# Attention with rotary embedding, then a gated MLP, on one core: new orders of work for the five engines, two buffers for v, and a rope table loaded in halves

## What is computed

```
q_rot, k_rot = rotate(q), rotate(k)          # x1*cos - x2*sin, x1*sin + x2*cos
scores = (1/sqrt(64)) * q_rot @ k_rot.T      # 576 x 576 for each of 32 heads
attn = exp(scores - max) / (sum + 1e-9)
x = attn @ v                                 # 2304 x 512 over all heads
h = x @ w_in                                 # 2304 x 2048
g = h * tanh(log1p(exp(min(h, 20))))
y = g @ w_out                                # 2304 x 512
```

## Time and profile before

| what | value |
|---|---|
| median of three runs | 646.28 us (643.45 to 646.46) |
| the profiled execution's own time | 643.55 us |
| its span (first to last instruction) | 641.8 us |
| busy in the span: PE, ACT, DVE, POOL | 95%, 67%, 52%, 40% |
| Vt of the last pair, the end of attention on PE | from 241.70 us for 0.72 us |
| mean granted TensorE clock | 0.995 of full speed |

### The profile page before, as it was taken

The page is one execution under the profiler, slowest core; times in us unless marked ns, Lnnn a source line. Parts: engine busy times, 40 slices in busy tenths (PEclk is TensorE's granted clock), DMA queues, the critical chain, the costliest instruction groups (busy, mean ns, idle before and its releaser), DMA issues.

```text
span 641.8 us, 12510 instructions
## 1 busy us (share of the span) xinstructions
PE 610.3 (95%) x4484; PEld 467.2 (73%) x4484; DVE 331.4 (52%) x541; ACT 429.4 (67%) x693; POOL 259.6 (40%) x210
## 2 busy tenths in 40 slices
PE   0699999999999989999999999999999999999998
PEld 0366666666666658978888888888888888888886
DVE  1567777677778763864433335333534335234331
ACT  1567878788787766575865748675488575586663
POOL 3976778777878346996000431000620006000000
PEclk9989999999999989999999999999999999999999
DMA  6757786677777625050000051000330000000001
GB/s 217 206 168 195 212 239 198 187 221 222 209 204 197 168 63 151 1 131 34 0 1 1 0 132 66 1 0 2 93 103 0 0 0 0 33 33 0 0 0 65
DMA packets 39343, 60.20 MB, mean 94 GB/s; under 512 B 4880, under 2 KB 25104, under 8 KB 39184
## 3 DMA queue, kind: packets, MB, share of 16 engines
q1 hardware_dynamic: 39312, 59.79, 31.9%
HBM read 43.19 MB, written 9.51 MB: 82 GB/s over the span
## 4 chain that ended last, share of the span: by engine, by line
PE 82%; POOL 7%; DMA 5%; SPq 3%; issue 1%; DVE 1%; ACT 1%; ACTq 0%; POOLq 0%; DVEq 0%
PE ps_s L639 10%; PE ps_y L809 10%; PE ps_y L810 10%; PE ps_y L811 10%; PE ps_t L715 10%; PE ps_h L785 9%; PE ps_h L786 9%; PE ps_h L787 9%; PE ps_t L667 5%; POOL raw L504 2%; DMA xb_l<-r_early 2%; PE ps_t L727 1%; DMA raw<-qk_in 1%; POOL wout_lo L581 1%; DMA v_st<-v_in 1%
## 5 line engine op out<-in xcount | busy, mean ns | idle before, releaser
L1103 DVE TENSOR_TENSOR h_sb<-h_sb,m_sb 128x1024 f32<-128x1024 f32 x36 | 56.4, 1568 | 145.5 <-ACT m_sb L956 145.5
L1022 DVE TENSOR_SCALAR_CACHE_REDUCE minus_s<-ps_s 128x576 f32<-128x576 f32 x144 | 105.3, 753 | 34.1 <-PE ps_s L639 31.9
L809 PE MATMUL ps_y<-wout_hi,gh 128*128 128x512 f32 x288 | 112.2, 390 | 1.5 <-POOL wout_lo L581 1.5
L810 PE MATMUL ps_y<-wout_lo,gh 128*128 128x512 f32 x288 | 112.1, 389 | 0.0
L811 PE MATMUL ps_y<-wout_hi,gl 128*128 128x512 f32 x288 | 112.1, 389 | 0.0
L639 PE MATMUL ps_s<-qk_b,qk_a 64*128 64x288 f32 (+1 forms) x320 | 95.2, 442 | 15.7 <-DMA qk_b<-qk_a 12.2
L876 ACT ACTIVATE prob<-minus_s,neg_max 128x576 f32<-128x576 f32 x128 | 98.2, 774 | 13.6 <-DVE minus_s L1022 13.3
L504 POOL TENSOR_TENSOR raw<-raw,rope_t 128x576 f32<-128x576 f32 x62 | 86.7, 1421 | 50.2 <-DMA raw<-qk_in 50.2
L785 PE MATMUL ps_h<-xb_h,win_hi 128*128 128x512 f32 x256 | 99.6, 389 | 0.0
L786 PE MATMUL ps_h<-xb_l,win_hi 128*128 128x512 f32 x256 | 99.6, 389 | 0.0
L787 PE MATMUL ps_h<-xb_h,win_lo 128*128 128x512 f32 x256 | 99.6, 389 | 0.0
(11 more groups left out here) (71 smaller groups left out, 1018.4 us busy)
## 6 DMA issues: line engine op xcount, KB each, us to landing
raw<-qk_in SPq DMA_DIRECT2D x32, 576.0 KB, 4.1
v_st<-v_in SPq DMA_DIRECT2D x32, 160.0 KB, 2.3
qk_b<-qk_a SPq DMA_DIRECT2D x32, 144.0 KB, 2.4
x_transposed<-xt SPq DMA_DIRECT2D x64, 72.0 KB, 2.1
y_out<-y_sb SPq DMA_DIRECT2D x18, 256.0 KB, 2.0
win_raw<-w_in SPq DMA_DIRECT2D x16, 256.0 KB, 4.4
wout_raw<-w_out SPq DMA_DIRECT2D x16, 256.0 KB, 4.5
x_raw<-x_transposed SPq DMA_DIRECT2D x4, 1024.0 KB, 5.6
```

The costliest lines, as they stand in the source:

```text
L809: nc.tensor.matmul(o, g_h, wout_hi[:, f, :], start=(f == 0), stop=False)
L810: nc.tensor.matmul(o, g_h, wout_lo[:, f, :], start=False, stop=False)
L1022: nc.vector.tensor_scalar(minus_s[:, ring(word)], ps_s[:, score_buf(word, m), :, 0:SIDE], -1.0, None, ALU.mult, ALU.min, accum_out=neg_max ...
L1103: nc.vector.tensor_tensor(h_sb[:, c % 2, :], h_sb[:, c % 2, :], m_sb[:, c % 2, :], ALU.mult).then_inc(g_mul, 1)
```

## The change

Five things change together.

1. The three lists of words are new. On PE the four V words stand apart, each between scores, ST comes behind S0b, and TQ and Vt stand last. ACT and DVE follow this order.
2. `TURN_PAIR`: G4 moves to the pair of banks of V, and G0a and G1a to the other.
3. v has two buffers, so `load_v` of pair n waits for Vt of pair n-2 only, and v of pair 0 is loaded before the first step.
4. The rope table is loaded in two DMAs, one for each head, and DVE waits for the first alone.
5. In POOL's step `rotate(1, n + 2)` moves ahead of `add_parts(0, n + 2)`. Because ST is now behind S3a, `add_parts(0, ...)` waits for ST of pair n instead of S3a.

```diff
-PE_STEP = "S0a ST V0- V1- G4- S1a G0b- S2a S3a G1b- V2- V3- S0b S1b TQ Vt- S2b S3b G0a G1a".split()
-ACT_STEP = "G4- S0a G0b- ST G1b- S1a S2a S3a Xa- Xb- TQ S0b G0a G1a S1b S2b S3b".split()
-DVE_STEP = "S0a ST G4- S1a G0b- S2a G1b- S3a S0b S1b TQ S2b S3b G0a G1a".split()
+PE_STEP = "S0a S1a G4- G0b- S2a V0- S3a S0b G1b- V1- ST S1b G0a V2- S2b G1a S3b V3- TQ Vt-".split()
+ACT_STEP = "G4- S0a G0b- S1a S2a G1b- S3a S0b G0a ST S1b G1a S2b S3b Xa- Xb- TQ".split()
+DVE_STEP = "S0a G4- S1a S2a G0b- S3a S0b G1b- ST G0a S1b S2b G1a S3b TQ".split()
...
-TURN_PAIR = {"V": 0, "G4-": 1, "G0b-": 1, "G1b-": 1, "TQ": 1, "G0a": 0, "G1a": 1}
+TURN_PAIR = {"V": 0, "G4-": 0, "G0b-": 1, "G1b-": 1, "G0a": 1, "G1a": 1, "TQ": 1}
...
-        v_st = sb1("v_st", [P, 2, NT, D])
+        v_st = sb1("v_st", [P, 2, 2, NT, D])
...
-            def load_v(e, p):
+            def load_v(e, p, m):
...
-                if due(p):
-                    sp.wait_ge(pv_done, p)
+                if due(p - 1):
+                    sp.wait_ge(pv_done, p - 1)
                     sp.sem_inc(sp_through, 1)
-                sp.dma_start(v_st[:, e, :, :], head).then_inc(v_loaded[e], 16)
+                sp.dma_start(v_st[:, m, e, :, :], head).then_inc(v_loaded[m][e], 16)
...
-                if real(n):
+                if real(n) and not (isinstance(n, int) and n == 0):
                     for e in range(2):
-                        load_v(e, n)
+                        load_v(e, n, m)
...
             load_raw(0, 0)
-            sp.dma_start(rope_t[:], rope).then_inc(rope_loaded, 16)
-            load_raw(1, 0)
+            for e in range(2):
+                sp.dma_start(rope_t[:, e], rope[:, e]).then_inc(rope_loaded[e], 16)
+                if e == 0:
+                    load_raw(1, 0)
...
             load_raw(1, 1)
+            for e in range(2):
+                load_v(e, 0, 0)
...
                 if real(n + 2):
+                    rotate(1, n + 2)
                     add_parts(0, n + 2, m)
                 if real(n - 1):
                     keep_sums(n - 1, 1 - m)
                 if real(n + 2):
-                    rotate(1, n + 2)
                     add_parts(1, n + 2, m)
...
-            dve.wait_ge(rope_loaded, 16)
+            dve.wait_ge(rope_loaded[0], 16)
```

More of the change, by code:

```diff
@@ L193, in sem @@
             return top.enter_context(nc.semaphore(name))
-        rope_loaded = sem("rope_loaded")
+        rope_loaded = [sem(f"rope_loaded_{e}") for e in range(2)]
         id_loaded = sem("id_loaded")
         raw_loaded = [sem(f"raw_loaded_{e}") for e in range(2)]
-        v_loaded = [sem(f"v_loaded_{e}") for e in range(2)]
+        v_loaded = [[sem(f"v_loaded_{m}_{e}") for e in range(2)] for m in range(2)]
         rope_parts = [sem(f"rope_parts_{e}") for e in range(2)]
@@ L498, in _ @@
         def _(pool):
-            pool.wait_ge(rope_loaded, 16)
+            for e in range(2):
+                pool.wait_ge(rope_loaded[e], 16)
             def rotate(e, p):
@@ L704, in x_part, with p_times_v @@
                 return ps_t[side * D:side * D + D, TURN_PAIR["V"], e, first:first + count]
-            def p_times_v(part, p):
+            def p_times_v(part, p, vm, loads):
                 e, half = part // 2, part % 2
@@ L711, in p_times_v @@
                     pe.wait_ge(tails_taken_a if e == 0 else tails_taken_v, p + 1)
-                    pe.wait_ge(v_loaded[e], 16 * (p + 1))
+                    pe.wait_ge(v_loaded[vm][e], 16 * loads)
                 for kt in (2 * half, 2 * half + 1):
                     for side in range(2):
-                        mm = nc.tensor.matmul(x_part(e, side, 0, SIDE), v_st[:, e, kt, :],
+                        mm = nc.tensor.matmul(x_part(e, side, 0, SIDE), v_st[:, vm, e, kt, :],
                                               pt[:, e, kt, side * SIDE:(side + 1) * SIDE],
@@ L718, in p_times_v, with ends_times_v @@
                 mm.then_inc(pt_read[e], 1)
-            def ends_times_v(p):
+            def ends_times_v(p, vm):
                 pe.wait_ge(ends_taken_a, p + 1)
@@ L726, in ends_times_v @@
                         rows = slice(e * D, e * D + D)
-                        mm = nc.tensor.matmul(x_part(e, side, first - side * SIDE, count), v_st[rows, e, 4, :],
+                        mm = nc.tensor.matmul(x_part(e, side, first - side * SIDE, count), v_st[rows, vm, e, 4, :],
                                               pt[rows, e if own else 0, 4, first:first + count],
@@ L730, in ends_times_v, with step @@
                 mm.then_inc(pv_done, 1)
-            def step(n, m):
+            def step(n, m, i):
                 for word in PE_STEP:
@@ L757, in step @@
                     elif word == "Vt-":
-                        ends_times_v(p)
+                        ends_times_v(p, 1 - m)
                     else:
@@ L761, in step @@
                             wait_turn_banks("V", n)
-                        p_times_v(int(word[1]), p)
+                        p_times_v(int(word[1]), p, 1 - m, i + m)
             for n in range(2 * LOOP[0]):
-                step(n, n % 2)
+                step(n, n % 2, n // 2)
             with pe.Fori(*LOOP) as i:
                 for m in range(2):
-                    step(2 * i + m, m)
+                    step(2 * i + m, m, i)
             for n in range(2 * LOOP[1], PAIRS + 1):
-                step(n, n % 2)
+                step(n, n % 2, n // 2)
             def hidden(b, c):
```

## The result

The changed kernel took **672.16 us** (median of 4 runs, 670.46 to 673.14) beside 646.10 for the kernel before (4 runs on the same chip, 643.45 to 646.46). The ratio is 1.041, 95% interval 1.0374 to 1.0446: slower by 4.1%. The sign was forecast, the size was not: 672.16 lies above the range of 648 to 668. The profiled execution is the one of 670.46 us, its span 668.7 against 641.8.

The account below looks back on a forecast made before the run. PE bound the kernel before; afterwards the ring through POOL would. Twelve rings of 14.7 us instead of 159.55 give +16.85, less 1.4 and 1.7: +13.75 on 643.55, 657.3, set at 658.5 for the median; range 648 to 668.

Parts of the forecast that it names:

- The ring of POOL, move and raw load: Add head a, move, raw load, multiply, weights, add again: 11.6 us before, forecast at 14.7 against a step of 13.30.
- all three waits: Forecast in each step: POOL for head a's raw load, ACT for POOL's COPY of sums, PE for ACT's copy of G0b.
- POOL's part: POOL's own work inside the ring, with head b's multiplications moved in: 4.68 + 2.75 + 1.41 = 8.84 us.
- Move to multiplication: Time from the start of head a's move on SP to POOL's multiplication of its raw data: taken as 5.9 us.
- the second ring: Not forecast: kept sums through ACT, PE, copy of x and SP's stores to the move, which it delays 0.7 to 1.1 us.
- the second rival: The ring binds, but with fast loads: ring of 13.9 us, about 649 us in all; chance 0.12.
- the third rival: PE's waits lower TensorE's clock in each step's V words, delaying stores and next move: about 666 us; chance 0.12.
- The start: Exponentials of S0a for pair 2 come 1.4 us earlier than before, 0.6 for the halved rope table included.
- The end: After pair 14 PE sets the pace: 0.83 for v and about half the last step's waits, -1.7 us together.
- PE's words: PE alone needs about 13.1 us a step: 0.43 of waits gone, 0.1 for each of two added switches.
- the first rival: Faster: the ring stays hidden under PE's 13.1 us, 7.7 us gained together, about 637 us; chance 0.08.
- v in two buffers: Removes PE's two waits for v, 4.3 us: 0.83 gained at the end, the 3.5 in step 1 gaining nothing in itself.

Follow-up runs that it names:

- the COPY ahead: The changed kernel with keep_sums moved ahead of head b's multiplications, which stay ahead of head a's sum: 664.07 us, ratio 1.0273.

## Why the prediction was right in kind and too small

It is settled at the end of Vt of the last pair, in the profiled executions: 269.53 against 242.42, 27.1 us later, where +13.75 was forecast. (The prediction takes 241.70 for the end of Vt; it is the start, which does not touch the sum.) The MLP behind it is unchanged, as forecast.

- **What binds: right.** PE bound the kernel before, by little. The ring of POOL, move and raw load, and the way from the kept sums by ACT to PE, show in all three waits, and that one moved call cost 23.4 us in the kernel before and 29.7 in the changed one.
- **POOL's part: right.** 8.84 forecast, 8.83 measured.
- **Move to multiplication: the term that was mis-sized first.** "I therefore take 5.9, near the slow end", and 6.36 was measured in the mean of 12, close to the slowest of the 11 rows. 0.46 in 12 steps are 5.5 us. The reason given fits the run that holds head b's transfers back (5.38). The value was a fair reading of the rows at hand: in the five of the 11 in which head b's move followed within 2.26 to 2.54 us, the load took 5.47 to 6.49, 5.91 in the mean. But none of them has the 1.86 of the changed kernel. A value from the old range of distances was carried over to one outside of it. In the kernel before with POOL's new order, where the distance is 1.8 to 1.9 too, the load takes 6.32.
- **The stores and the second ring: the step that failed in substance.** The ring was summed as if the move could always go when head a's sum is done. "The stores ... speak against a ring this short" was used against the second rival only, and their price was left out of the sum. They cost 3.5 us by the rows, 5.1 by the run without them. They come late because PE comes late, so this ring passes through PE and its clock. In the kernel before with the new order of POOL they hold up no move, so this price belongs to the order together with the new words.
- **The clock: the third rival was part of the truth.** It had 0.12 and a place of its own, yet here it came along with the forecast's ring and not in its place. PE waited about 2 us every other step, and the V word behind the wait took 2.19 instead of 1.19. The lower clock does not follow from a ring that is too long: with POOL's new order in the kernel before, and with the COPY ahead, PE waited in almost every step and the clock from 50 to 200 us was 0.99. Against this rival stood that the waits of the kernel before had left the clock alone; those were of tenths of a microsecond in most steps, so they were weak evidence. The Trainium skill (TensorE: Matmul & The Clock Gate, section "HAM oscillation — how this bites in real kernels") describes kernels that wait in every round and are throttled anew in each. The changed kernel agrees with it from 80 us on, with 0.50 to 0.65 granted in the 3 us behind its longer waits; the two runs just named, which wait in almost every round and are hardly throttled, do not. What the clock costs by itself was not separated from the stores and the sums; no run did this. POOL's order cost 6.3 us more in the changed kernel (29.7) than in the kernel before (23.4), where the clock stayed up, and that holds the stores and all else that differs. 666 was its price in the forecast, still 6 too low, since neither the slower load nor the reciprocals were in it.
- **DVE's reciprocals: missed.** They were not moved by the change and not looked at. They wait for a COPY that the change makes late; 2.2 us by the rows (221.83 - 204.18 = 17.65 for step 13, against 15.47 for a ring), 2.8 to 8.7 by the run.
- **The start: -1.4 forecast, -0.3 measured.** The first COPY of the sums started at 48.30, where 47.8 was forecast: the halves of the rope table did nothing for POOL (its first multiplication started at 9.63, and at 8.79 before), though DVE began at 5.89 and not 7.28. No run tried the halves alone, so the 0.6 taken for them stays without one. The exponentials then waited for DVE until 48.94.
- **The end: -1.7 forecast, -1.0 measured.**
- **PE's words: 13.1 us forecast, 13.42 measured** where PE alone binds. The "0.43 us a step" of waits went, as forecast, but the two added switches, with the rest of the new order, cost some 0.55 and not 0.2; 0.3 of it is in the V words. With 13.42, the first rival's sum gives 641.7 and not 637 (0.12 lost in 14 steps instead of 0.2 gained), and the run with POOL's old order, which is that case, took 642.43.
- **v in two buffers: right for this kernel, and a trap.** "I gain nothing in itself" in step 1 because POOL binds; with POOL's old order it is the one part of the change that pays, 5.4 us. "PE has no wait for v" was not borne out: one of 2.6 us is left in an early step.

Summed up: of the 13.4 missing at the last Vt, the time from move to multiplication gives 5.5, stores 3.5, reciprocals 2.2, start and end 1.8; 0.4 is not placed. These are readings of the rows of one execution. The runs bear out each part's sign and about its size, but they don't add up one by one, since each part shortens a ring of which another link then comes last.

**What stays open.** The clock's own share, and why long and short steps take turns. How much of the slower load of head a is head b's transfers and how much the weights behind them. And whether the raw load issued ahead of the move, which would take some 1.4 us of issue out of the ring, brings the new order of POOL back under PE's step; it was not tried.

## What to carry to other kernels

Before an operation is moved on an engine with idle time, look for the ring that passes through it (a buffer, its load, the queue that issues the load) and compare the whole ring with the step: here an engine idle for 3 us a step had 1.7 us to spare, and 2.75 moved into the ring cost 23 to 30 us. A ring that comes out longer than the bound engine's step costs about the difference in every step (22.4 of 23.4 us in the kernel before). It can cost more, as here in the changed kernel: the bound engine waits, may get a lower clock, delivers late, and so delays the stores that stand in the same queue ahead of the ring's own transfers. A transfer's time is to be read from rows with the new distance to its neighbours, or taken as a range beyond the slowest row. A change of several parts is best split: one buffer gave the whole gain here, and one moved call lost four to six times as much.

## What was not expected of the hardware

- A wait of only 2.1 to 2.2 us on TensorE was followed by a granted clock of 0.58 over 3 us, in steps in which PE was otherwise busy all the time. It is not a matter of the wait alone: in the changed kernel waits of 1.89 and 1.80 us were followed by 1.00, and with the COPY ahead a wait of 2.21 (before 181.75) by 1.00 and one of 2.05 (before 197.29) by 0.61.
- Head b's move and load, started 1.9 us behind head a's of the same size by one queue, with the weights and v behind them, delayed head a's by 1.0 us (5.38 to 6.36), though the mean DMA share of the stretch is 0.66, below the 0.72 of the kernel before (100 to 150 us in both). The mean share told nothing of the delay. Over the whole kernel the median from issue to landing of a raw load rose from 4.1 to 5.2 us, and that of v from 2.3 to 5.4, as it is now issued right behind the others.
- Splitting V into four words costs 0.15 us in the V words for each added switch between V and scores, with no wait in it, and the new order some 0.55 a step in all.
